# Two-layer gated network behind windowed attention: the layer's last two groups in one second product, and three orders of issue changed

## The reference

```python
# attention: 4 batches, 8 heads, 576 positions, head size 64, window of 128
scores = scale * np.matmul(q, k.transpose(0, 1, 3, 2))
scores = np.where(mask, scores + bias[None], -1000000000.0)
attn = softmax(scores)                       # over the last axis
x = (attn @ v), heads side by side           # 2304 tokens x 512
x = (sigmoid(x @ w_gate) * (x @ w_val)) @ w_out      # d_ff 1536
x = ((x @ w1) * (x @ w2) @ w3) @ w_out2              # d_ff 1024
```

## Time and profile before

| | us |
|---|---|
| median of 3 runs | 1018.2 (1017.22 to 1023.16) |
| the profiled execution, device time | 1019.72 |
| its span, first to last instruction | 1017.9 |
| PE busy | 919.8 |
| GpSimd (POOL) busy | 737.3 |
| DVE busy | 602.1 |
| ACT busy | 549.9 |
| mean granted TensorE clock (1 is 2.4 GHz) | 0.971 |
| chain that ended last: PE | 71% |
| chain that ended last: POOL | 13% |

### The profile page before, as it was taken

The page is one execution under the profiler, slowest core; times in us unless marked ns, Lnnn a source line. Parts: engine busy times, 40 slices in busy tenths (PEclk is TensorE's granted clock), DMA queues, the critical chain, the costliest instruction groups (busy, mean ns, idle before and its releaser), DMA issues.

```text
span 1017.9 us, 16149 instructions
## 1 busy us (share of the span) xinstructions
PE 919.8 (90%) x5352; PEld 855.0 (84%) x5352; DVE 602.1 (59%) x1364; ACT 549.9 (54%) x1259; POOL 737.3 (72%) x626
## 2 busy tenths in 40 slices
PE   3899798999996999978999997799987999987998
PEld 2676587999995899878998996799977999977998
DVE  4657564566666555644665657465574555684555
ACT  4657576666674654446665774565534344334330
POOL 3657998877866986678778775877856877749750
PEclk9999998999998999989999999999998999998999
DMA  6334222323121311042221221122104211112101
GB/s 204 120 104 153 74 96 81 99 89 99 49 82 37 101 62 57 24 148 80 94 83 60 68 76 49 63 92 74 48 10 156 83 63 63 62 42 83 63 21 63
DMA packets 46050, 80.81 MB, mean 79 GB/s; under 512 B 4112, under 2 KB 27280, under 8 KB 45968
## 3 DMA queue, kind: packets, MB, share of 16 engines
q1 hardware_dynamic: 45968, 79.77, 23.4%
HBM read 72.94 MB, written 6.82 MB: 78 GB/s over the span
## 4 chain that ended last, share of the span: by engine, by line
PE 71%; POOL 13%; DVE 7%; issue 4%; DMA 2%; ACT 1%; SPq 1%; DVEq 0%; POOLq 0%; ACTq 0%
PE quad_ps L576 13%; PE quad_ps L578 12%; PE quad_ps L577 12%; PE o_ps L576 8%; PE o_ps L578 7%; PE o_ps L577 7%; POOL wq_lo L1290 2%; PE attn_ps L599 2%; PE attn_ps L576 2%; PE attn_ps L614 2%; POOL xs_lo L1254 2%; DMA wo_lo_raw<-w_out 2%; POOL wq_lo L1283 1%; POOL soft L1239 1%; DVE xf L1072 1%
## 5 line engine op out<-in xcount | busy, mean ns | idle before, releaser
L576 PE MATMUL quad_ps<-xs_hi,wq_hi 128*128 128x384 f32 x840 | 296.8, 353 | 36.4 <-POOL wq_lo L1290 17.8
L578 PE MATMUL quad_ps<-xs_hi,wq_lo 128*128 128x384 f32 x840 | 287.7, 342 | 0.0
L577 PE MATMUL quad_ps<-xs_lo,wq_hi 128*128 128x384 f32 x840 | 287.2, 342 | 0.0
L576 PEld LDWEIGHTS quad_ps<-xs_hi,wq_hi 128*128 128x128 f32 x840 | 163.0, 194 | 44.3 <-POOL wq_lo L1290 19.8
L576 PE MATMUL o_ps<-h_hi,wo_hi 128*128 128x384 f32 x480 | 167.0, 348 | 10.5 <-DVE xf L1072 10.0
L577 PEld LDWEIGHTS quad_ps<-xs_lo,wq_hi 128*128 128x128 f32 x840 | 163.1, 194 | 0.0
L578 PEld LDWEIGHTS quad_ps<-xs_hi,wq_lo 128*128 128x128 f32 x840 | 162.1, 193 | 0.0
L578 PE MATMUL o_ps<-h_hi,wo_lo 128*128 128x384 f32 x480 | 161.5, 337 | 0.0
L577 PE MATMUL o_ps<-h_lo,wo_hi 128*128 128x384 f32 x480 | 161.3, 336 | 0.0
L1021 DVE TENSOR_TENSOR u<-quad_ps,s 128x384 f32<-128x384 f32 x60 | 33.5, 558 | 196.6 <-PE quad_ps L578 195.2
L1290 POOL TENSOR_TENSOR wq_lo<-wsum,wq_hi 128x1024 fp32r<-128x1024 f32 x60 | 143.5, 2392 | 7.7
(11 more groups left out here) (91 smaller groups left out, 1807.4 us busy)
## 6 DMA issues: line engine op xcount, KB each, us to landing
raw_q<-w SPq DMA_DIRECT2D x24, 512.0 KB, 3.5
raw_q<-w_gate SPq DMA_DIRECT2D x18, 512.0 KB, 3.5
raw_q<-w_val SPq DMA_DIRECT2D x18, 512.0 KB, 4.5
wo_lo_raw<-w_out SPq DMA_DIRECT2D x18, 512.0 KB, 3.5
wo_lo_raw<-w_times_wout SPq DMA_DIRECT2D x12, 512.0 KB, 3.7
w_raw<-w3t SPq DMA_DIRECT2D x16, 256.0 KB, 2.7
q_lo_raw<-qT SPq DMA_DIRECT2D x16, 192.0 KB, 3.8
bias<-bias SPq DMA_DIRECT2D x12, 256.0 KB, 4.5
```

The source lines that it names most:

```text
L576: pe.matmul(out, lh, rh, start=start, stop=False, skip_group_check=onto)
L577: pe.matmul(out, lh, rl, start=False, stop=False, skip_group_check=onto)
L578: return pe.matmul(out, ll, rh, start=False, stop=stop, skip_group_check=onto)
```

## The change

1. **One product section for a layer's last two groups.** `SECTIONS` names the last two product sections of a layer pair0 and pair1. Both handle the last two groups (4 and 5, 8 and 9 of a pass): tiles 0 to 3 in pair0, 4 to 7 in pair1, each tile accumulated over both groups in its PSUM bank and added into xf once. A tile order `O_TILES` that begins with tokens' second half comes with it, and new counts (`tiles_to`, `WHOLE`) in the waits of all engines. The number of sections stays.
2. **The orders around it.** DVE's and ACT's work in pair0 and pair1: x_sum and x_lo of P5 move forward, ACT rounds P3 before P7. In the last gate section of a pass DVE makes x_sum(P5).
3. **GpSimd's order.** In a layer's first val section plain_lo and sums_lo of the next group come first; out_lo comes behind weight_sums. In pair1 the four low parts of x follow soft.
4. **The head.** PE's slot is scores, fold, turn, fold, pv, and the last folds go into slots 33 to 36. v_hi and w_hi move from DVE to ACT. w3 is loaded into three buffers of half a block, two slots earlier, in the place of xt1 and xt2.
5. **A third softmax buffer**: score(n) waits for turn(n-3) instead of turn(n-2), and for exp(n-2).

The diff, cut to its core (the same for soft[n % 3] and for the names of the w3 buffers in the other lines):

```diff
-FOLDS_IN = [[k for k in range(NFOLD - IB) if fold_slot(k) == s] for s in range(SLOTS)]
-W3_LOAD_SLOT = {1 + 2 * h: h for h in range(2, HALVES)}
+FOLDS_IN = [[k for k in range(NFOLD) if fold_slot(k) == s] for s in range(SLOTS + 1)]
+W3_LOAD_SLOT = {2 * h - 1: h for h in range(3, HALVES)}
...
 SECTIONS = []
+PROJECTS = []
 for g_ in range(NG):
-    SECTIONS += [(g_, "gate", g_), (g_, "val", g_)]
-    if not first_of(g_):
-        SECTIONS.append((g_, "proj", g_ - 1))
+    SECTIONS += [(g_, "gate"), (g_, "val")]
     if last_of(g_):
-        SECTIONS.append((g_, "proj", g_))
+        SECTIONS += [(g_, "pair0"), (g_, "pair1")]
+        PROJECTS.append((g_ - 1, g_))
+    elif not first_of(g_):
+        SECTIONS.append((g_, "proj"))
+        PROJECTS.append((g_ - 1,))
 PASS_SECTIONS = len(SECTIONS) // NPASS
...
+def project_of(g):
+    return [e for e, groups in enumerate(PROJECTS) if g in groups][0]
+def tiles_to(g):
+    return 8 * (project_of(g) + 1) if g >= 0 else 0
...
-        O_TILES = [(0, 0), (0, 1), (1, 0), (1, 1), (1, 2), (1, 3), (0, 2), (0, 3)]
-        WHOLE = {P1: 2, P5: 4, P6: 6, P7: 6, P3: 6, P2: 8, P4: 8}
+        O_TILES = [(1, 0), (1, 1), (0, 0), (0, 1), (1, 2), (1, 3), (0, 2), (0, 3)]
+        WHOLE = {P1: 4, P5: 4, P6: 6, P7: 6, P3: 6, P2: 8, P4: 8}
...
+            def project(e, k, g):
+                start, stop = g == PROJECTS[e][0], g == PROJECTS[e][-1]
+                c, o = O_TILES[k]
+                t, hb = 8 * e + k, g % 2
                 if k == 0:
                     pe.wait_ge(wo_split, g + 1)
-                    if g == 0:
+                    if e == 0:
                         pe.wait_ge(fold_copied, IB)
-                c, o = O_TILES[k]
-                t, hb = 8 * g + k, g % 2
                 pe.wait_ge(h_split, 4 * g + 1 + max(HALF_OF[0][c], HALF_OF[1][c]))
-                wait(pe, acc_done, t - 1)
+                if start:
+                    wait(pe, acc_done, t - 1)
                 for f in range(FG):
                     w = slice(f * DM + o * P, f * DM + (o + 1) * P)
                     hp = piece(HALF_OF[f][c])
                     mm = product(ps_o[t % 2][:, 0:TH], (wo_hi[hb][:, w], wo_lo[hb][:, w]),
-                                 (h_hi[hb][:, hp], h_lo[hb][:, hp]), start=f == 0, stop=f == FG - 1)
-                mm.then_inc(o_done, 1)
+                                 (h_hi[hb][:, hp], h_lo[hb][:, hp]), start=start and f == 0, stop=stop and f == FG - 1)
+                if stop:
+                    mm.then_inc(o_done, 1)
...
             for s in range(SLOTS):
+                if 0 <= s - LAG_QK < HEAD:
+                    scores(s - LAG_QK)
+                for k in FOLDS_IN[s][0:1]:
+                    fold(k)
+                if 0 <= s - LAG_TURN < HEAD:
+                    turn(s - LAG_TURN)
+                for k in FOLDS_IN[s][1:2]:
+                    fold(k)
                 if 0 <= s - LAG_PV < HEAD:
                     pv(s - LAG_PV)
-                if 0 <= s - LAG_TURN < HEAD:
-                    turn(s - LAG_TURN)
-                for k in FOLDS_IN[s]:
-                    fold(k)
-                if 0 <= s - LAG_QK < HEAD:
-                    scores(s - LAG_QK)
-            for k in range(NFOLD - IB, NFOLD):
+            for k in FOLDS_IN[SLOTS]:
                 fold(k)
...
+                    e = project_of(g - 1)
+                    if kind == "proj":
+                        parts = [(k, g - 1) for k in range(8)]
+                    else:
+                        lo = 4 * (kind == "pair1")
+                        parts = [(lo + k, of) for k, of in ((0, g - 1), (1, g - 1), (0, g), (1, g),
+                                                            (2, g - 1), (3, g - 1), (2, g), (3, g))]
+                    for i, (k, of) in enumerate(parts):
+                        project(e, k, of)
+                        if i == 1 and m is not None:
+                            turn(m)
+                        if i == 5 and m is not None:
...
+                if s in W3_HI_SLOT:
+                    hf = W3_HI_SLOT[s]
+                    act.wait_ge(w3_in[hf % 3], 16 * (hf // 3 + 1))
+                    wait(act, fold_half, hf - 1)
+                    nc.scalar.copy(w3_hi[:, w3_cols(hf)], w3_raw[hf % 3][:, :]).then_inc(w3_hi_done, 1)
+                for j in range(HEAD_JOBS):
+                    if s == FIRST[j] + 6:
+                        values_hi(j)
...
-                wait(dve, turned, n - 1)
+                wait(dve, turned, n - 2)
+                wait(dve, exp_done, n - 1)
...
+                elif kind == "pair0":
+                    hidden(g, C21)
+                    hidden_lo(g, C21)
...
+                    add_up(e, 0)
+                    add_up(e, 1)
+                    if more and g % GP == GP - 1:
+                        x_lo(inst, P5)
+                    add_up(e, 2)
+                    add_up(e, 3)
...
+                elif g % GP == G1 - 1:
                     x_sum(inst, P5)
...
+                    x_lo(inst, P5)
+                    add_up(e, 4)
+                    add_up(e, 5)
...
+                elif kind == "val" and first_of(g):
+                    plain_lo(g + 1, 0)
+                    sums_lo(g + 1, 0)
+                    if n is not None:
+                        normalise(n)
+                    weight_sums(g + 1, 1)
+                    splits(sec)
+                    out_lo(g)
+                    plain_lo(g + 1, 1)
```

220 lines of the change are left out of this document (101 added, 119 removed).

## The result

The changed kernel takes 1075.3 us (median of 4 runs, 1075.1 to 1075.5), the kernel before 1019.3 beside it: 1.0545 times as long, 95% interval 1.0511 to 1.0578. I had said 1027, at most 1042.

A forecast was written before the change was run, and what follows sets the result against it. TensorE, busy 919.8 of 1017.9 us, was taken as the bound, leaving its idle 98 us and the clock to change. Head +36.8, GpSimd's order -5 and pairs -23 made +8.8: 1027.0 us, 8-in-10 range 1001 to 1042.

The forecast's parts named there:

- Head, +36.8: Everything before the first gate section: 24.6 us of added waits, 5.2 of clock and 7 at its end.
- Clock +5.2: In the head, three more stretches at low granted clock behind waits above 4 us, 1.75 us each; bounds 0 and 17.
- GpSimd by first use, -5: Val0 and gate1: gate1's 4.6 us wait goes, put-off work comes slightly late; net -5 us, bounds -8 and 0.
- B: Change of layer after group 9, no attention: waits for xf and most of gate11's wait go, -5 us.
- E: Change of layer after group 25, no attention: gate27 comes earlier, val27 2.0 us late, -7.5 us.
- A: Change of layer after group 5, with attention: pair1 waits 3.7 us, gate7's wait for wq_lo goes, net -2 us.
- C: Change of layer after group 15, with attention: pair1 waits 2.7 us, gate17's 4.1 us wait goes, -4 us.
- D: Change of layer after group 19: pair1 starts 2.1 us late, waits for xf of 5.0 go, -4.5 us.
- second rival: In the pairs, DVE's conversions meet GpSimd's wq_lo, two per change of layer, each 1 us longer: +10, 1037 us; 18%.
- Pairs -23: The shared second product at the five changes of layer gives back TensorE idle time: -23 us, bounds -40 and 0.
- third rival: The pairs give nothing since the waits of 7.0 and 6.61 us remain, -5 instead of -23: 1045 us; 7%.
- first rival: The head isn't held up because v_hi comes in time, costing 0 to 7 us there: 993 us; 15%.

The follow-up runs named there:

- head-back kernel: Changed kernel with TensorE's head slot back to pv, turn, folds, scores and v_hi, w_hi back on DVE: 1026.9 us.
- mended kernel: Head-back kernel with put-off work placed by due time, k_lo and q_lo before weight_sums, x_sum(P5) in pair0, x_lo(P5) behind tile 4's addition: 992.5 us.

## Why the prediction was wrong

**Head, +36.8; measured +41.6.** The chain and its main places were right: 4.6, 4.1 and 4.6 before the scores of slots 10, 17 and 24 were 4.5, 3.9 and 4.8, and slot 20's 4.3 for w_lo was 3.8. The five slots that I gave 11.9 came to 9.0, and the longest of these waits, 3.1, is released by DVE's negmax in the trace. Three terms were mis-sized and partly cancelled, so that the head came within 5 us was luck: against the head-back kernel, which has the third buffer too, it is 50.9 us later.
- "The third softmax buffer: 0" was -9.3 (5.5 to 9.3 by the traces). I saw that score would no longer wait for the turn, and dismissed it because DVE then waits for pt_hi; but pt_hi of that step is done a slot before, and v_hi, w_hi and GpSimd behind them move up. I had worked out w_lo's lateness slot by slot and not asked why DVE's v_hi was late.
- "Clock +5.2" was 12.8 in busy time. I counted three slow stretches more than before, behind waits above 4 us; the granted clock fell to 0.57 behind the wait of 1.85 too, and stayed at 0.50 through most of the tail.
- "Filling the tail costs 6.5", behind turn(26), was 11.7: from turn(26) at 151.72 to val0 33.5 us, 21.9 before (my own times, 28.2 against 21.1, made 7.1 of it). No run takes the tail alone, but with v_hi and w_hi on DVE the same stretch is 26.2, so scores first is 4.3 of it and ACT's part 7.3; 4.4 of the 11.7, ahead of the first gate section, are clock.

Up to turn(26) the head is 29.9 us longer; from 26 us on TensorE is idle 21.6 us more there, where I had 25.1, and busy 8.4 more.

**"GpSimd by first use, -5"; as built about +13.** This step and the next but one failed most, by 18 and 19 us. I did list what is put off and found it 1 us late for val1, but I left out of that list the instructions that wait for it on other engines: ACT's second part of wq_hi, which stands in ACT's queue ahead of h_hi and s, and k_lo and q_lo, which TensorE needs at the first step of a job. And I did the list once, for val0, while the order holds at all six places; at B and E I reckoned with the put-off wq_lo alone, at A and C with nothing.

**"x_sum(P5) in the last gate section": not priced; +6 at D.** The list of the change names this edit, my sum does not. It is the second rival's mechanism (DVE's conversions held by GpSimd), at a place where I had not looked: I looked in the pairs, and gave it 1 us for each conversion, outside the sum. In its place x_sum(P5) took 5.04 for 0.95 and held score.

**"Pairs -23".** A to E came out +12.6. Of that 10.2 is GpSimd's order (7.0 + 5.0 + 0.3 + 0.8 - 2.9) and 6 is x_sum(P5); what is left for the pairs is some -4, and -1.2 by the run without pairs, where the orders were mended on both sides. The sizes at the first stop were right: pair1 of A waits 3.48 (said 3.7), C's 2.36 (2.7), D's 2.37 (a delay of 2.1), B's two pair sections last 18.0 us. What was wrong is that the rest of the idle time would go. The turn in gate6 waits 4.0 instead of 7.0, but pair1 is 3 us longer; TensorE's wait for sig, which stands in ACT's queue behind the load of w_out, is 5.2 at B and at D. That fewer additions are no gain where a chain of conversions is the bound fits these waits; no run varies the additions alone.

The signs that I had named nearly all came in: the three waits in the head, val0 near 180, no wait for wq_lo, 3.48 and 2.36 in pair1 of A and C, 18.0 for B's pair. They stood only where the prediction had looked. In the window that I had read A is 1.6 us shorter; followed on to the end of val7 it is 5.9 longer, and "an A that is longer" was my sign of being wrong.

The 48 us between 1027 and 1075 are thus 23 - 4 = 19 from the pairs, 5 + 13 = 18 from GpSimd's order, 6 from x_sum(P5) and 5 from the head, to within a microsecond or two. The third rival (1045, at 7%) was the nearest on the pairs: it gave them -5. The second (1037) had a mechanism that is there, but not at its place: the addition behind x_lo(P5) made TensorE wait 3.48 us at most, under its 4, and where DVE's wait for GpSimd cost most was D. The first rival (993) failed on TensorE's waits; that the total can be as low is shown by the 992.5 of the mended kernel, by another way.

## What to carry to other kernels

When an in-order engine's work is reordered by first use, what is put off must be placed by its own due time, and that is the moment at which any queue on any engine stands behind its result, not the moment at which TensorE reads it. Before pricing an edit that removes a wait at 0, ask what stands behind the waiting instruction: here that line was worth 6 to 9 us, the largest gain in the change as built. Name signs of being wrong behind the stretch that an edit touches, not only in it. And a mixed change should be taken apart before it is thrown away: of this one the third buffer, the pairs and the orders, once mended, make the kernel 2.7% faster than before (992.5 us), while two conversions moved to ACT cost 43.6, and 26 of that came back when they stood ahead of a copy.

## What was unexpected of the hardware

A DVE instruction with two inputs in SBUF can be held by more than one GpSimd instruction. x_sum(P5) started 0.2 us behind wo_lo, was passed over by wo_lo and by three wsum that followed each other without a gap (784.39 to 788.83), and ended 0.8 us after the third of them. The fourth, which waits for the third's semaphore and began 0.07 us behind it, in turn took 1.32 us for 0.72. Elsewhere in the same trace the instruction gets in behind the first, as in the earlier trace rows: an xs_lo from 356.28 to 358.21 is held by one that ends at 357.40. The Trainium skill, SBUF — State Buffer, "Who interferes with whom", has the lock held for a whole instruction and the loser blocked. The two runs at this place agree with a lock (0.95 us when GpSimd waits, 5.04 beside it), but a row of instructions held it here, and what decides who gets it between two of them I did not try.

The granted clock, over a head with ten waits of 1.4 to 7 us, was 0.80 where the same work without most of them had 1.00. The same window, from 26 us to the first gate section, in the head-back kernel:

```profile
26.00:123.34 97.34, 89.35 (x559) 68.82 (x559) 66.68 (x206) 68.78 (x236) 78.56 (x86) 1.00 0.36 113
```

TensorE was busy 107.4 us for what took 89.4. Of the 48.8 us between these two windows 18 are clock, so more than a third of the loss was not waiting.
